# Moving a group of on-chip tiles by some hundred bytes in a fused attention, MLP and mixture-of-experts kernel

## The chip, the cores and the metric

The kernel runs on one core of a Trainium2 chip. The metric is the device time of one execution in microseconds (us). The engines are named as in the profile: PE is TensorE (matmul), PEld its weight loads, DVE is VectorE, ACT is ScalarE, POOL is GpSimd, and SP is SyncE, which issues most transfers.

## The reference, cut to what matters

Three stages follow one another. Sizes: 8 batches, 8 heads, 512 rows and 32 state rows of 64 values per head; so 8 x 544 = 4352 tokens of 512 values reach the MLP.

```python
def _attn_ref(x, state):                       # x (8, 8, 512, 64), state (8, 8, 32, 64)
    a = softmax(scale * x @ state.T)           # rows read the state
    xread = a @ state
    a2 = softmax(scale * state @ x.T)          # the state reads the rows
    sread = a2 @ x
    return concat([xread, sread], axis=2)

def _moe_ref(x, w_in, w_out):                  # (512, 2048), (2048, 512)
    h = x @ w_in
    return (h * clip(h + 3, 0, 6) / 6) @ w_out

def _moe2_ref(x, w_gate, w_output_gate, w1, w2):   # 8 experts, 512 -> 1024 -> 512
    e = argmax(x @ w_gate); gate = softmax(x @ w_gate)[e]
    eom = sigmoid(x @ w_output_gate)[e]
    out = gate * eom * (relu(x @ w1[e]) @ w2[e])   # each token by its one expert
```

## The kernel before, in words

Matmuls keep close to fp32 precision by three products: each operand is split into a high part of type fp32r (ScalarE copies it) and the rest (VectorE subtracts), and high x high, high x low and low x high are summed.

First half, until about 680 us. For each of eight batches, a block runs 16 steps of the MLP: L837 makes one 128 x 512 tile of the hidden layer from the attention weights (`att1_hi`, `att1_lo`, in the profile `att_hi` and `att_lo`) and a product of state and `w_in` that is made beforehand (`mix`); ScalarE and VectorE apply the activation; L855 multiplies by `w_out`, whose output stays in four PSUM banks. Between these steps stand the attention of the next batch (L776 scores, L785 transposes, L796 the read of `xb` with the weights `att2_t`) and the choice of expert of the batch before it; tables written out by hand (`ATT`, `POST`, `MIX`) fix their places. Rows are scattered to a bucket of their expert in HBM. A ninth, shorter block does the state's tokens (L827).

Second half. A loop goes over tiles of 128 rows from the buckets: rows are loaded to `xg`, turned by VectorE to `xg_raw` and split to `xg_t`; L912 multiplies by `w1`; ScalarE puts the result in `expert_hid`, which is written to `hidden` in HBM (L601) and read back in another order to `hid_mv` (L609), turned and split to `act_t`; L928 multiplies by `w2`; VectorE scales the result into `yo`, and GpSimd scatters it to the output (L691). When the expert changes, the next expert's raw weights, 2 MB each, which ScalarE's queue loads to `raw1` and `raw2` (L1119, L1125), are split into the half of `we` that isn't in use (L1076 on ScalarE, L483 on VectorE). The order of work on each engine is fixed by the program; waits are on semaphores.

Memory is laid out by hand. `at(name, offset, shape, dtype)` places a tile at `SBUF_BASE + offset` bytes of every partition, with `SBUF_BASE = 16512`. A running offset `o` is increased after each group, and many tiles lie over others whose time has passed. The order, from offset 131072 on, is: `mix` (16384 bytes), `hid_hi` with its followers and `att1_lo` (16384), `rows` at 163840, `keys0` (2048), `xb` (8192), `x_t` with `att2_t` (8192), then `late_at`: `sc1` (4096), `att1_hi` (4096), `att2` (4096), `sread` (4096), `keys1` (2048), `wg`, `ident`, two constants of type bf16, and then small tiles. In the second half the first 131072 bytes hold `we`, 131072 holds `raw2`, 147456 `act_t`, 163840 `xg` and `hid_mv` (over `rows`), and these lie behind it:

```python
    raw1_at = 163840 + ROWS_SIZE + 2048
    raw1 = at("raw1", raw1_at, [P, KD * F], F32)
    assert raw1_at + KD * F * 4 == late_at
    expert_hid = at("expert_hid", late_at, [P, F], F32)
    xg_t = [at(f"xg_t_{n}", late_at + 8192 + i * 4096, [P, 2, KD, P], F32R) for i, n in enumerate(("hi", "lo"))]
    yo = [at("yo0", raw1_at - 2048, [P, DM], F32), at("yo1", st_diag_at, [P, DM], F32)]
```

`st_diag_at` is the offset of `keys1`. P is 128 and BANK is 512; `rows` has CH x ROW = 4 x 516 values of 4 bytes a partition, 8256 bytes.

Of the kernel before, what the change touches and what calls it, by code (L numbers as in the profile page):

```python
# [25 lines left out]
F32 = mybir.dt.float32  # L26
# [7 lines left out]
P = 128  # L34
BANK = 512
# [4 lines left out]
def emit_kernel(nc, x_rows, x_t_dram, keys, w_in, w_out, gates, w1, w2, out):  # L40
# [4 lines left out]
    E = w1.shape[0]  # L45
    F = w1.shape[3]
    SCALE = float(D) ** -0.5
    KD = DM // P
    KF = FF // P
    KE = F // P  # L50
    CH = S // P
# [8 lines left out]
    ROW = DM + 4  # L60
# [16 lines left out]
    def at(name, offset, shape, dtype):  # L77
        return nc.alloc_sbuf_tensor_at(name, shape, dtype, offset=SBUF_BASE + offset)
# [4 lines left out]
    o = 131072  # L83
# [21 lines left out]

    x_t_second = at("x_t_second", 65536 + 2 * GO * DM * 4, [P, PAIRS, S], F32)

    ROWS_SIZE = -(-CH * ROW * 4 // BANK) * BANK
    o += ROWS_SIZE

    half_b = B // 2
# [30 lines left out]
    keys_s.append(at("keys1", o, [P, half_b, PAIRS, NS], F32))  # L142
    o += 2048

    wg = at("wg", o, [P, KD, 4 * E], F32)
    o += 512
    ident = at("ident", o, [P, P], F32)
    o += 512
    before = at("before", o, [P, P], BF16)
# [5 lines left out]
    def sb(name, shape, dtype=F32):  # L155
        n = 1
        for s in shape[1:]:
            n *= s
        size = -(-n * (2 if dtype == BF16 else 4) // 32) * 32
        small[0] += size  # L160
        assert small[0] <= 212832, small[0]
        return at(name, small[0] - size, shape, dtype)
# [90 lines left out]
    gate_s = sb("gate_s", [P, RING, ROW - DM])  # L253
    raw1_at = 163840 + ROWS_SIZE + 2048
    raw1 = at("raw1", raw1_at, [P, KD * F], F32)
# [1387 lines left out]
```

## Time and profile before

| | us |
|---|---|
| three runs | 1160.65, 1162.46, 1165.16 |
| median | 1162.46 |
| the profiled execution | 1165.16 |
| its span, first to last instruction | 1163.3 |
| mean granted TensorE clock, of full speed | 0.985 |

The profile is of one execution. Busy time of an engine is the time in which it had an instruction under way. The chain that ended last is followed back from the last instruction, at each step to what released it. In the windows view a DMA share of 1.00 means that all 16 DMA engines were busy throughout.

### The profile page before, as it was taken

To read this page: it belongs to the slowest core of one execution; us is meant where nothing else is said; L and a number is where in the kernel's file an instruction comes from. 1 tells how busy PE (TensorE), PEld (TensorE's weight loads), DVE (VectorE), ACT (ScalarE), POOL (GpSimd) and SP (SyncE) were. 2 spreads that over 40 slices of the span, in tenths; PEclk is the share of its full clock that TensorE was granted. 3 is DMA by queue.
4 is the path that set the end of the run, shared out by engine and by line. 5 is a ranking of instruction groups with operands and counts; after the bars stand their busy time and mean duration, and the time that the engine had idled before them with its cause. 6 is when DMAs were issued, how large, how long until landed. Compare 5 with 4: busy or idle time off the path is not lost.

```text
span 1163.3 us, 20895 instructions
## 1 busy us (share of the span) xinstructions
PE 1121.6 (96%) x6358; PEld 887.2 (76%) x6359; DVE 639.1 (55%) x1247; ACT 467.1 (40%) x780; POOL 77.0 (7%) x96
## 2 busy tenths in 40 slices
PE   9999999999999999999999988989999999979995
PEld 7777777777777777777778977767888888858884
DVE  6675654655646556556564347546474445556632
ACT  4554434443444344434544351425343223344420
POOL 0000100101001001010010110010110010101111
PEclk9999999999999999999999989999999999989998
DMA  9210111102101111020020275667675444847542
GB/s 366 90 37 7 67 37 37 43 32 74 37 6 69 37 37 41 33 74 1 1 110 1 101 245 179 217 237 233 203 248 180 153 145 130 282 149 215 161 139 65
DMA packets 98783, 131.36 MB, mean 113 GB/s; under 512 B 13967, under 2 KB 75023, under 8 KB 94352
## 3 DMA queue, kind: packets, MB, share of 16 engines
q1 hardware_dynamic: 91360, 89.35, 24.3%
q10 hardware_dynamic: 1584, 23.07, 5.5%
q0 software_dynamic: 5760, 17.90, 4.0%
q8 instruction: 47, 0.77, 0.3%
q14 instruction: 32, 0.26, 0.1%
HBM read 85.86 MB, written 45.47 MB: 113 GB/s over the span
## 4 chain that ended last, share of the span: by engine, by line
PE 85%; DVE 4%; DMA 3%; issue 3%; ACTq 2%; ACT 1%; SPq 1%; DVEq 0%; POOL 0%; POOLq 0%
PE y_ps L855 33%; PE h_ps L837 15%; PE y_ps L928 13%; PE y_ps L912 7%; PE h_ps L912 6%; PE a_ps L812 2%; PE h_ps L827 2%; DMA hidden<-expert_hid 1%; DMA hid_mv<-hidden 1%; ACTq L444 1%; DVE we L483 1%; PE a_ps L715 1%; PE a_ps L796 1%; SPq L609 1%; PE a_ps L776 1%
## 5 line engine op out<-in xcount | busy, mean ns | idle before, releaser
L855 PE MATMUL y_ps<-w_out_hi,hid_hi 128*128 128x512 f32 x544 | 217.6, 400 | 0.0
L855 PE MATMUL y_ps<-w_out_hi,hid_lo 128*128 128x512 f32 x544 | 212.2, 390 | 0.0
L855 PE MATMUL y_ps<-w_out_lo,hid_hi 128*128 128x512 f32 x544 | 212.0, 390 | 0.0
L928 PE MATMUL y_ps<-we,act_t_hi 128*128 (+1 forms) x608 | 189.0, 392 | 6.2 <-DVE act_t_lo L1559 3.6
L1365 DVE SCALAR_TENSOR_TENSOR hid<-hid,h_ps 128x512 f32<-128x512 f32 (+1 forms) x144 | 94.5, 656 | 166.3 <-ACT hid L1035 164.7
L837 PE MATMUL h_ps<-att_hi,mix 128*128 128x512 f32 x512 | 184.0, 402 | 0.1
L1035 ACT ACTIVATE hid<-h_ps,three 128x512 f32<-128x512 f32 (+1 forms) x144 | 95.5, 663 | 174.8 <-PE h_ps L837 151.4
L855 PEld LDWEIGHTS y_ps<-w_out_hi,hid_hi 128*128 128x128 f32 x544 | 102.1, 188 | 49.9 <-issue 30.4
L928 PEld LDWEIGHTS y_ps<-we,act_t_hi 128*128 128x128 f32 x608 | 114.6, 189 | 31.9 <-issue 8.2
L1374 DVE TENSOR_TENSOR hid_lo<-hid,hid_hi 128x512 fp32r<-128x512 f32 (+1 forms) x144 | 94.9, 659 | 70.5 <-ACT hid_hi L1043 69.5
L1552 DVE STREAM_TRANSPOSE act_raw<-hid_mv 128x512 f32<-128x512 f32 x76 | 49.5, 690 | 136.2 <-DMA hid_mv<-hidden 134.8
L855 PEld LDWEIGHTS y_ps<-w_out_hi,hid_lo 128*128 128x128 f32 x544 | 102.1, 188 | 22.3
L928 PE MATMUL y_ps<-we,act_t_lo 128*128 (+1 forms) x304 | 118.8, 391 | 0.0
L855 PEld LDWEIGHTS y_ps<-w_out_lo,hid_hi 128*128 128x128 f32 x544 | 102.3, 188 | 19.6
L837 PEld LDWEIGHTS h_ps<-att_hi,mix 128*128 128x128 f32 x512 | 96.1, 188 | 27.4 <-issue 7.0
L1043 ACT ACTIVATE hid_hi<-hid 128x512 fp32r<-128x512 f32 (+1 forms) x144 | 87.4, 607 | 67.0 <-DVE hid L1365 66.8
L912 PE MATMUL h_ps<-we,xg_t_hi 128*128 (+1 forms) x304 | 96.1, 398 | 9.9 <-DVE we L483 8.2
L912 PE MATMUL y_ps<-we,xg_t_hi 128*128 x304 | 95.2, 395 | 8.8 <-DVE xg_t_lo L1419 8.8
L837 PE MATMUL h_ps<-att_lo,mix 128*128 128x512 f32 x256 | 99.9, 390 | 0.0
L483 DVE TENSOR_TENSOR we<-raw,we 128x1024 f32 (+1 forms) x55 | 63.9, 1220 | 30.9 <-ACT we L1076 30.7
L1113 ACT ACTIVATE act_t_hi<-act_raw 128x512 fp32r<-128x512 f32 x76 | 45.8, 630 | 84.2 <-DVE act_raw L1552 84.1
L912 PEld LDWEIGHTS h_ps<-we,xg_t_hi 128*128 128x128 f32 x304 | 58.2, 192 | 23.1 <-issue 11.0
(216 smaller groups left out, 1409.5 us busy)
## 6 DMA issues: line engine op xcount, KB each, us to landing
raw<-in_w ACTq DMA_DIRECT2D x11, 2048.0 KB, 8.4
hidden<-expert_hid SPq DMA_DIRECT2D x76, 256.0 KB
hid_mv<-hidden SPq DMA_DIRECT2D x152, 128.0 KB
xg<-buckets SPq DMA_DIRECT2D x164, 64.0 KB
xb<-in_x_rows SPq DMA_DIRECT2D x8, 1024.0 KB, 4.9
x_t<-in_x_t SPq DMA_DIRECT2D x7, 1024.0 KB, 4.9
buckets<-pad_row SPq DMA_DIRECT2D x8, 774.0 KB, 8.0
raw<-in_w SPq DMA_DIRECT2D x3, 2048.0 KB, 7.5
```

What stands on the lines that cost most here:

```text
L483: ins = eng.tensor_tensor(we[:, bass.ds(w_at + piece(w, i, LO), PIECE)], raw[:, i * PIECE:(i + 1) * PIECE], we[:, bass.ds(w_at + piece(w, ...
L812: i = pe.matmul(mix_bank(a, n, g)[NS * q:NS * q + NS, :], keys_of(a)[D * g:D * g + D, q, :], w_in_raw[D * g:D * g + D, q, mix_columns(n)], ...
L837: i = pe.matmul(h_ps[:, j % 2, 0:cols], mix[:, m % SLOTS, g, n % GO, wp, :], (att1_hi, att1_lo)[tp][:, g, 0:cols], start=(g == 0 and k == ...
L855: i = pe.matmul(y_ps[:, t, :], (hid_hi, hid_lo)[hp][:, hid_at(b, j), t * P:(t + 1) * P], w_out_s[wp][:, j, :], start=(j == 0 and m == 0), ...
L912: i = pe.matmul(hid2_banks[slot % 2][:, h, :], xg_t[xp][:, slot % 2, k, :], we[:, bass.ds(w_at + (wp * WPART + k * F + h * BANK), BANK)], ...
L928: i = pe.matmul(y2_ps[:, slot % 2, :], act_t[hp][:, slot % 2, f, :], we[:, bass.ds(w_at + (wp * WPART + KD * F + f * DM), DM)], start=(f = ...
L1035: act.activation(hid[:, hid_at(b, j), 0:cols], h_ps[:, j % 2, 0:cols], ACT.Relu, bias=three).then_inc(sem("relu_ready"), 1)
L1043: act.activation(hid_hi[:, hid_at(b, j), 0:cols], hid[:, hid_at(b, j), 0:cols], ACT.Copy).then_inc(sem("hid_hi_ready"), 1)
L1113: act.activation(act_t[HI][:, slot % 2, h * 4:h * 4 + 4, :], act_raw[:, slot % 2, h * 4:h * 4 + 4, :], ACT.Copy).then_inc(sem("act_t_hi"), 1)
L1365: dve.scalar_tensor_tensor(out=hid[:, hid_at(b, j), 0:cols], in0=hid[:, hid_at(b, j), 0:cols], scalar=6.0, in1=h_ps[:, j % 2, 0:cols], op0 ...
L1374: dve.tensor_tensor(hid_lo[:, hid_at(b, j), 0:cols], hid[:, hid_at(b, j), 0:cols], hid_hi[:, hid_at(b, j), 0:cols].bitcast(F32), ALU.subtr ...
L1552: dve.transpose(act_raw[:, slot % 2, h * 4:h * 4 + 4, :].rearrange("p f t -> p (f t)"), hid_mv[:, h, :, :].rearrange("p s (k f) -> p k s f ...
```

## The change

The room behind `rows` is rounded up to a multiple of 128 bytes, 8320, where it was rounded to a multiple of 512, 8704. `wg` is placed 512 bytes further from the running offset, and the offset behind it grows by 1024 where it grew by 512. No instruction, loop, wait or transfer is added, taken away or put in another order.

```diff
-    ROWS_SIZE = -(-CH * ROW * 4 // BANK) * BANK
+    ROWS_SIZE = -(-CH * ROW * 4 // P) * P
     o += ROWS_SIZE
...
-    wg = at("wg", o, [P, KD, 4 * E], F32)
-    o += 512
+    wg = at("wg", o + 512, [P, KD, 4 * E], F32)
+    o += 1024
     ident = at("ident", o, [P, P], F32)
```

## Rows read from the trace of the kernel before

**Rows 1.** Part 1 of the page: busy us, share of the span, instructions.

```profile
PE 1121.6 (96%) x6358; PEld 887.2 (76%) x6359; DVE 639.1 (55%) x1247; ACT 467.1 (40%) x780; POOL 77.0 (7%) x96
```

**Rows 2.** Part 4 of the page: the chain that ended last, by engine.

```profile
PE 85%; DVE 4%; DMA 3%; issue 3%; ACTq 2%; ACT 1%; SPq 1%; DVEq 0%; POOL 0%; POOLq 0%
```

**Rows 3.** Windows of stages: busy us and count, granted clock, DMA share, GB/s.

```profile
60.00:600.00 540.00, 540.00 (x3312) 407.18 (x3311) 314.00 (x659) 238.86 (x417) 27.88 (x28) 1.00 0.12 41
...
695.00:830.00 135.00, 120.97 (x621) 99.41 (x620) 78.98 (x147) 48.11 (x71) 9.88 (x10) 0.96 0.66 213
830.00:985.00 155.00, 155.00 (x686) 128.38 (x685) 76.19 (x126) 51.59 (x83) 13.70 (x15) 1.00 0.56 175
985.00:1030.00 45.00, 36.78 (x156) 30.04 (x155) 28.97 (x41) 18.77 (x26) 3.90 (x4) 0.92 0.64 211
```

**Rows 4.** The chain in order of time (start us, us, what): start and busy stages.

```profile
1.05 5.54 PE h_ps L876 x60
...
93.03 2.96 PE y_ps L855 x12
95.99 2.72 PE h_ps L837 x12
100.96 2.72 PE y_ps L855 x12
...
822.61 5.44 PE h_ps L912 x24
828.05 5.44 PE y_ps L928 x24
```

**Rows 5.** The chain in order of time, around two changes of expert.

```profile
by line: PE y_ps L855 32.6%; PE h_ps L837 15.2%; PE y_ps L928 13.1%; PE y_ps L912 7.2%; PE h_ps L912 6.4%; issue 2.6%; PE a_ps L812 2.5%; PE h_ps L827 2.0%; DMA hidden<-expert_hid 1.5%; DMA hid_mv<-hidden 1.3%; ACTq L444 1.2%; DVE we L483 1
...
752.48 0.35 ACTq L1119
...
759.10 0.34 ACTq L1125
...
762.43 9.52 DMA hidden<-expert_hid
...
1002.24 0.34 ACTq L1125
...
1005.37 7.42 DMA hidden<-expert_hid
```

**Rows 6.** Windows of single transfers: x_t, raw1, expert_hid out (850 to 852), hid_mv (854).

```profile
466.50:467.00 0.50, 0.50 (x4) 0.42 (x3) 0.50 (x1) 0.00 (x0) 0.00 (x0) 1.00 1.03 426
467.00:467.50 0.50, 0.50 (x4) 0.42 (x3) 0.14 (x1) 0.32 (x1) 0.00 (x0) 1.00 0.97 410
...
584.00:585.00 1.00, 1.00 (x6) 0.83 (x5) 1.00 (x2) 1.00 (x3) 0.00 (x0) 1.00 0.99 426
585.00:586.00 1.00, 1.00 (x6) 0.84 (x5) 1.00 (x3) 0.27 (x1) 0.00 (x0) 1.00 1.07 459
...
850.00:851.00 1.00, 1.00 (x6) 0.81 (x5) 1.00 (x4) 0.44 (x1) 0.00 (x0) 1.00 0.70 262
851.00:852.00 1.00, 1.00 (x6) 0.84 (x5) 1.00 (x2) 0.00 (x0) 0.00 (x0) 1.00 0.68 258
...
854.00:855.00 1.00, 1.00 (x6) 0.84 (x5) 0.58 (x1) 0.00 (x0) 0.00 (x0) 1.00 1.06 358
```

**Rows 7.** Instructions of L796 and L837: ns least/median/most, first and last start us.

```profile
L796 PEld LDWEIGHTS a_ps<-xb,att_t x512: 106/110/110, 42.2 to 541.6; 128*32 128x32 f32 x171
L796 PE MATMUL a_ps<-xb,att_t x512: 219/219/243, 42.2 to 541.6; 128*32 128x64 f32 x171
...
L837 PE MATMUL h_ps<-att_hi,mix x512: 388/389/499, 18.7 to 625.5; 128*128 128x512 f32 x171
...
L837 PE MATMUL h_ps<-att_lo,mix x256: 387/389/398, 19.0 to 625.3; 128*128 128x512 f32 x128
```

## The prediction

> **What bounds the kernel now.** I read the page's busy shares first, then the chain that ended last, then windows of single stages. TensorE is busy 96% of the span and VectorE, the next one, 55% [rows 1]; the chain gives TensorE 85% of the span, DMA 3% [rows 2]. The windows show that these are two different regimes: from 60 to 600 us and from 830 to 985 us TensorE has no idle time at all, while around two changes of expert it does: 135 - 120.97 = 14.0 us idle between 695 and 830 us, and 45 - 36.78 = 8.2 us between 985 and 1030 us [rows 3]. In the busy stages the chain is a run of matmuls at an even pitch: 12 in 2.72 us in the first half, 24 in 5.44 us in the second, 227 ns each in both [rows 4]. So a change matters if it alters that pitch, or if it alters the transfers that the chain runs through at the changes of expert [rows 5].
>
> **What the edit moves.** It changes addresses alone: the same instructions in the same order with the same waits, bytes and semaphores. The sum over removed and added instructions is therefore 0 and what is left is whether an address has a price. `rows` takes 8256 bytes a partition; its room shrinks from 8704 to 8320, so everything from `keys0` to `keys1` moves down by 384 bytes. `wg` then gets a hole of 512 bytes ahead of it, so that it and all behind it move up by 128. Start addresses: `keys0` goes from 16512 + 163840 + 8704 = 189056, which is 738 x 256 + 128, to 188672 = 737 x 256. `wg` goes from 225920 (882 x 256 + 128) to 226048 = 883 x 256. Before, every large tile starts 128 bytes past a multiple of 256. After, those ahead of and including `rows` still do, and those behind it start on a multiple of 256. Aliased tiles keep their places relative to one another: `raw1` still ends at `late_at`, and `xg` with `hid_mv` (8192 bytes) still end ahead of `yo0`, 128 bytes away where it was 512. No new overlap, hence no new wait.
>
> **Its parts.** (1) Transfers with a moved end: the loads of `x_t`, `xb`, `keys`, `wg` and `raw1`, the writes of `expert_hid` to HBM, and the stores of `yo`. The other end is in HBM and stays. `raw2`, `xg`, `hid_mv` and the scattered `rows` stay. (2) TensorE operands that move: `att1_hi` (streamed by 512 matmuls on the chain of the first half), `xg_t` (only as weights), and the small ones `x_t`, `xb`, `att2_t`, `ident`, `wg`. All operands of L855 and L928, the largest groups, stay. (3) Operands of VectorE and ScalarE in the attention and in the split of `w1`.
>
> Part 1, from the DMA windows. Bandwidth divided by the busy share is what the 16 DMA engines reach when all are busy. The load of `raw1` (runs of 16 KB a partition) reaches 426/0.99 = 430 and 459/1.07 = 429 GB/s; the load of `x_t` (runs of 8 KB) 426/1.03 = 414 and 410/0.97 = 423; the write of `expert_hid` (runs of 2 KB) 262/0.70 = 374 and 258/0.68 = 379; a stretch of mostly 512-byte runs 358/1.06 = 338 [rows 6]. With 377 GB/s a 2 KB run takes 2048 / (377/16) = 87 ns of one engine, with 430 a 16 KB run takes 610 ns. A line through both has 0.0365 ns a byte and 12 ns fixed per run. Whatever a misplaced start costs per run is inside those 12 ns. If all of it vanished, 2 KB runs would be 14% faster and 16 KB runs 2%. That is the bound of the gain. Where is it exposed? The chain has 1.5% on the writes of `hidden`, and two pieces of it, 9.52 and 7.42 us, hold 16.9 us [rows 5]. 14% of 16.9 is 2.4 us. These pieces are far longer than 256 KB need (about 0.7 us at 377 GB/s): just before each, ScalarE's queue has issued the 2 MB load of `raw2` (L1125, at 759.10 and 1002.24), and before the first also that of `raw1` (L1119, at 752.48) [rows 5]. At 430 GB/s 2 MB take 4.9 us, so most of both pieces is the time of a load whose place is not changed (`raw2`) or can gain 2% (`raw1`, 0.1 us). What really belongs to `expert_hid` are its two writes of 0.7 us: 14% of 1.4 us is 0.2. So 2.4 is generous, and 0.3 us is nearer. The loads of `x_t` and `xb` inside the blocks lie under a TensorE without idle time [rows 3], and the first load of `x_t` lies under the 60 warm-up matmuls on which the chain stands until 6.59 us [rows 4]. Nothing. Stores of `yo` lie behind the matmuls until the very last, one of 256 KB: 14% of 0.7 us is 0.1. Part 1: between -2.5 us and 0, taken as -0.3.
>
> [...] No run here shows aligned runs yet.
>
> Part 2. The nearest rows are those where one line already starts at different residues. In L796 the weights are 32-column slices of `att2_t`, 128 bytes apart, so the 512 loads start 128, 256, 384 and 0 bytes past a multiple of 512 in turn. They take 106/110/110 ns (least, median, most). The streamed slices of `xb` are 256 bytes apart and take 219 ns at least and in the median [rows 7]. So the whole spread that an address could hide there is 4 ns. `att1_hi` and `att1_lo` both take 389 ns in the median in L837 [rows 7]. After the change they start at different residues. At 4 ns for each of the 512 matmuls on `att1_hi` the bound is 2.0 us lost; the same 4 ns the other way would be 2.0 gained, but the pitch of 227 ns is shared by forms with every kind of operand [rows 4], so I see nothing to gain. I take 0. Weight loads of `xg_t` run beside the matmuls (PEld 76% where PE has 96% [rows 1]) and would lie under them even 4 ns longer.
>
> Part 3. VectorE at 55% and ScalarE at 40% [rows 1] are not on the chain in the busy stages; at the changes of expert they are, with some dozens of instructions whose addresses partly moved. By the same 4 ns that is under 0.5 us either way. I take 0.
>
> **Sum.** The profiled execution took 1165.16 us, 1163.3 of span and 1.9 around it; with -0.3 it would take 1164.9. It was the slowest of three, 2.7 above the median of 1162.46. On the median: 1162.2 us. The bounds of the terms give -3.0 to +2.5.
>
> **Rivals.** A: start addresses matter to the DMA engines, and the changes of expert shorten. For it speak the chain's 16.9 us on `hidden` and the fixed part per run; against it that 16 KB runs already move at 430 GB/s from the old address, and that the same stalls hold waits on ScalarE and VectorE which don't move. At its bound it gives 1162.5 - 2.5 = 1160.0 us. To be faster by 0.5% (5.8 us) it would have to take a third off those 16.9 us, more than the 12 ns allow, unless a shorter transfer also gets a hidden write ahead of a 2 MB load; one such step, 7.42 us, would give 1155.0. B, the other side: TensorE reads `att1_hi` more slowly once it stands at another residue than the tiles that the other engines use at that time. Its place is L837 in the eight blocks, with no idle time under it to absorb it. For it speaks only that today all large tiles share one residue, so the trace can't show a mixture of them; against it the even spreads of L796, where slices at all four residues mix. It decides from 5.8 us / 512 = 11 ns a matmul, 5% of the pitch; at 15 ns it gives 1162.5 + 7.7 = 1170.2 us. C: a change of expert falls otherwise by chance, as transfers and queues shift by some tenths, and a stall grows or shrinks by one or two us. It gives 1160.5 to 1164.5, on either side.
>
> **Chances.** Within 0.5% (about what a measurement of this kernel can tell from no change; 1156.6 to 1168.3 us) lie my forecast at 0.68, C at 0.14 and A at or under its bound at 0.08: 0.90. A with a step ahead of a load, beyond 0.5%: 0.05. B beyond its threshold: 0.05. The range takes the lowest and highest of the three runs, 1160.65 and 1165.16, and adds the bounds of the terms, -3.0 and +2.5: 1157.6 to 1167.7.
>
> **What would show it.** Right: 12 matmuls of L837 still 2.72 us, both its forms at 389 ns, the write of `expert_hid` still near 377 GB/s at full share, the same instruction counts, the same idle time at the two changes of expert within 2 us. A: that rate at 400 or above and the pieces on `hidden` shorter. B: `att_hi` matmuls above `att_lo` and blocks longer than before. Wrong altogether: any group of VectorE or ScalarE whose mean moved by more than some ns.

## The result, and the profile after

Nine runs of each kernel: before 1165.16 us in the median (1160.65 to 1167.40), after 1172.17 us. The ratio is 1.0064, with a 95% interval of 1.0042 to 1.0087: slower by 7.5 us. One run of the changed kernel, 1598 us at a granted clock of 0.65, is left out of the ratio as disturbed; the other eight lie between 1167.90 and 1178.61. Four more executions of the changed kernel, the profiled one among them, took 1167.76, 1170.40, 1171.91 and 1173.89 us. The forecast was no change, 1162.2 us in a range up to 1167.7. The measured time lies above it. Of the 10.0 us between forecast and median, 2.7 are not the change: the kernel before had 1162.46 us in the median of its first three runs and 1165.16 in that of nine.

Order, counts, waits and transfers of the two kernels are the same, instruction for instruction. First the page of the changed kernel, its span, part 1 and the chain by engine, beside [rows 1, 2]:

```profile
span 1166.0 us, 20895 instructions
...
PE 1127.7 (97%) x6358; PEld 886.0 (76%) x6359; DVE 639.4 (55%) x1247; ACT 466.8 (40%) x780; POOL 76.8 (7%) x96
...
PE 85%; DVE 4%; issue 3%; DMA 2%; SPq 2%; ACTq 2%; ACT 1%; DVEq 0%; POOL 0%; POOLq 0%
```

VectorE, ScalarE and GpSimd are within 0.3 us of before. TensorE is busy 1127.7 - 1121.6 = 6.1 us longer with the same 6358 matmuls. That is the first hint: the work costs more where nothing waits. Then the chain of the changed kernel in order of time (start us, us, what), beside [rows 4]:

```profile
96.25 2.75 PE h_ps L837 x12
...
101.25 2.75 PE y_ps L855 x12
...
174.39 2.75 PE h_ps L837 x12
...
252.52 2.75 PE h_ps L837 x12
...
811.34 5.84 PE y_ps L912 x24
...
861.38 5.46 PE y_ps L928 x24
866.84 5.59 PE h_ps L912 x24
872.43 5.46 PE y_ps L928 x24
877.89 5.59 PE y_ps L912 x24
...
988.35 5.60 PE y_ps L912 x24
```

24 matmuls of L912 take 5.59 us where they took 5.44, (5.59 - 5.44)/24 = 6.2 ns each. 24 of L928 take 5.46, hardly more. In the first half, a block lasts 252.52 - 174.39 = 78.13 us; before, the same two groups stood at 173.71 and 251.45, 77.74 us apart. In [rows 4] 12 matmuls of L837 took 2.72 us where they now take 2.75, and so did 12 of L855, although both operands of L855 stand where they stood. The granted clock is 1.00 in both kernels from 60 to 600 us and from 830 to 985 us, so it isn't the clock. One step closer, the timeline of single matmuls in one L912 group after the change:

```profile
866.68 0.64 PE L912 MATMUL h_ps<-we,xg_t_hi 128*128 x2
867.15 0.39 PE L912 MATMUL h_ps<-we,xg_t_lo 128*128 x1
867.38 0.62 PE L912 MATMUL h_ps<-we,xg_t_hi 128*128 x2
867.84 0.39 PE L912 MATMUL h_ps<-we,xg_t_lo 128*128 x1
868.07 0.64 PE L912 MATMUL h_ps<-we,xg_t_hi 128*128 x2
```

and the same group before:

```profile
865.96 0.62 PE L912 MATMUL h_ps<-we,xg_t_hi 128*128 x2
866.42 0.39 PE L912 MATMUL h_ps<-we,xg_t_lo 128*128 x1
866.64 0.62 PE L912 MATMUL h_ps<-we,xg_t_hi 128*128 x2
867.10 0.39 PE L912 MATMUL h_ps<-we,xg_t_lo 128*128 x1
867.32 0.62 PE L912 MATMUL h_ps<-we,xg_t_hi 128*128 x2
```

Six matmuls take 867.32 - 865.96 = 1.36 us before and 868.07 - 866.68 = 1.39 after. Nothing is idle between them. A matmul's duration is longer than the interval to the next start (389 against 227 ns before), so the records overlap. The durations moved too, by a little less: from 389 to 393 and 395 ns in the median for L912, and for `att_hi` in L837 from 389 to 393 while `att_lo` stayed at 388 to 389. The weight loads of both stayed at 188 ns. The interval between starts gives the whole cost.

Where the 7.5 us are, by these rows. 38 tiles with 24 matmuls of L912 and 24 of L928 give at most 38 x (0.15 + 0.02) = 6.5 us. The last group of the first half (L855 x18) starts at 683.90 us where it started at 680.77, 3.1 us later. Together that is 9.6 us, of which some lies under other waits at the changes of expert. In the two profiled executions the spans differ by only 2.7 us, since the stretch from the last group of L855 to the first full run of L912 (from 680.77 to 811.46 before, from 683.90 to 811.34 after) was 3.2 us shorter in the execution of after; from there to the end it took 2.8 us longer, and 3.1 - 3.2 + 2.8 = 2.7. Over the kernels below that have this stall it lies between 126 and 132 us, whether `xg_t` is moved or not. So a span of one execution can't settle a half per cent here, while intervals of the even stretches repeat to 0.01 us (five blocks in a row at 77.74 us before and at 78.13 after). Such intervals, added up by line over five blocks of the first half, put 0.33 of the 0.39 us a block behind matmuls of L855 and 0.06 behind those of L837; no other line changes.

### The profile page after: what moved, and what is told of

The parts are those of the page before. It is cut to its first block, busy times and chain, and to the rows that moved or that the text cites. A ratio compares the mean times of both kernels' runs of the same rounds, so it can differ in the third digit from the quotient of the medians.

```text
span 1166.0 us, 20895 instructions
## 1 busy us (share of the span) xinstructions
PE 1127.7 (97%) x6358; PEld 886.0 (76%) x6359; DVE 639.4 (55%) x1247; ACT 466.8 (40%) x780; POOL 76.8 (7%) x96
## 4 chain that ended last, share of the span: by engine, by line
PE 85%; DVE 4%; issue 3%; DMA 2%; SPq 2%; ACTq 2%; ACT 1%; DVEq 0%; POOL 0%; POOLq 0%
PE y_ps L855 33%; PE h_ps L837 15%; PE y_ps L928 13%; PE y_ps L912 7%; PE h_ps L912 6%; PE a_ps L812 2%; PE h_ps L827 2%; DMA hid_mv<-hidden 1%; ACTq L444 1%; DVE we L483 1%; PE a_ps L715 1%; PE a_ps L796 1%; PE a_ps L776 1%; DMA hidden<-expert_hid 1%; SPq L574 1%
## 5 line engine op out<-in xcount | busy, mean ns | idle before, releaser
L855 PE MATMUL y_ps<-w_out_hi,hid_hi 128*128 128x512 f32 x544 | 218.6, 402 | 0.0
L855 PE MATMUL y_ps<-w_out_lo,hid_hi 128*128 128x512 f32 x544 | 213.0, 392 | 0.0
L855 PE MATMUL y_ps<-w_out_hi,hid_lo 128*128 128x512 f32 x544 | 212.6, 391 | 0.0
L928 PE MATMUL y_ps<-we,act_t_hi 128*128 (+1 forms) x608 | 187.9, 390 | 4.4 <-issue 2.6
L837 PE MATMUL h_ps<-att_hi,mix 128*128 128x512 f32 x512 | 184.5, 403 | 0.1
L855 PEld LDWEIGHTS y_ps<-w_out_hi,hid_hi 128*128 128x128 f32 x544 | 102.1, 188 | 51.1 <-issue 30.4
L928 PEld LDWEIGHTS y_ps<-we,act_t_hi 128*128 128x128 f32 x608 | 113.9, 188 | 30.3 <-issue 6.1
L855 PEld LDWEIGHTS y_ps<-w_out_hi,hid_lo 128*128 128x128 f32 x544 | 102.2, 188 | 23.2
L928 PE MATMUL y_ps<-we,act_t_lo 128*128 (+1 forms) x304 | 118.6, 390 | 0.0
L855 PEld LDWEIGHTS y_ps<-w_out_lo,hid_hi 128*128 128x128 f32 x544 | 102.3, 188 | 20.0
L837 PEld LDWEIGHTS h_ps<-att_hi,mix 128*128 128x128 f32 x512 | 96.1, 188 | 27.8 <-issue 7.0
L912 PE MATMUL h_ps<-we,xg_t_hi 128*128 (+1 forms) x304 | 97.1, 401 | 8.6 <-DVE we L483 7.6
L912 PE MATMUL y_ps<-we,xg_t_hi 128*128 x304 | 96.9, 400 | 8.4 <-DVE xg_t_lo L1419 8.4
L837 PE MATMUL h_ps<-att_lo,mix 128*128 128x512 f32 x256 | 99.9, 390 | 0.0
L912 PEld LDWEIGHTS h_ps<-we,xg_t_hi 128*128 128x128 f32 x304 | 57.8, 191 | 23.0 <-issue 9.8
```

Source lines behind the costliest of these rows:

```text
L837: i = pe.matmul(h_ps[:, j % 2, 0:cols], mix[:, m % SLOTS, g, n % GO, wp, :], (att1_hi, att1_lo)[tp][:, g, 0:cols], start=(g == 0 and k == ...
L855: i = pe.matmul(y_ps[:, t, :], (hid_hi, hid_lo)[hp][:, hid_at(b, j), t * P:(t + 1) * P], w_out_s[wp][:, j, :], start=(j == 0 and m == 0), ...
L912: i = pe.matmul(hid2_banks[slot % 2][:, h, :], xg_t[xp][:, slot % 2, k, :], we[:, bass.ds(w_at + (wp * WPART + k * F + h * BANK), BANK)], ...
L928: i = pe.matmul(y2_ps[:, slot % 2, :], act_t[hp][:, slot % 2, f, :], we[:, bass.ds(w_at + (wp * WPART + KD * F + f * DM), DM)], start=(f = ...
```

## The experiments

The theory that I formed from the trace, T: while one matmul streams its moving operand, the weights of the next are loaded. The rows show the overlap: in the kernel before, the weights of the matmul that starts at 866.64 us load from 866.42 on, 188 ns long, and the matmul ahead of it starts at 866.42 too. By T, if the two start at the same address modulo some power of two, matmuls follow one another in 227 ns; if not, they take some ns more. Before the change all large tiles started 128 past a multiple of 256, so they always agreed (were in step). Afterwards `xg_t` (weights of L912) and `att1_hi` (streamed in L837) start on a multiple of 256, and their partners `we` and `mix` don't. That the two disturb each other while one streams and the other loads is my assumption behind T, which no trace here shows directly; the experiments below test the agreement of the starts. The ratios below are each to the kernel before on the same chip, with their 95% interval.

**One part of the change alone.** `keys0` to `keys1` move, `wg` and the small tiles don't.

```diff
-    ROWS_SIZE = -(-CH * ROW * 4 // BANK) * BANK
+    ROWS_SIZE = -(-CH * ROW * 4 // P) * P
-    wg = at("wg", o, [P, KD, 4 * E], F32)
-    o += 512
+    wg = at("wg", o + 384, [P, KD, 4 * E], F32)
+    o += 512 + 384
```

> Only keys0 to keys1 (with xg_t, att1_hi, expert_hid, raw1) move down by 384 bytes; wg, ident and all small tiles stand where they stood before the change. Theory T (a matmul is slowed when the weights that load and the operand that streams start at different residues of the address): all of the change's loss comes from this part, so 24 matmuls of L912 take 5.59 us instead of 5.44, L928 stays near 5.44 to 5.46, a block of the first half takes 78.1 us instead of 77.7, and the time is 1.005 to 1.008 of before. Rival W (the loss comes from wg, ident, ones and the small tiles): 24 of L912 in 5.44 us, time within 0.2% of before.

Measured: ratio 1.0048 (1.0031 to 1.0065). L912 at 5.59 us, L928 at 5.46, two groups of L837 at 174.54 and 252.68 us, 78.14 apart. The intervals are those of the whole change, so W falls: `wg`, `ident` and the small tiles aren't the cause. The ratio ends just below what was expected; its interval overlaps with that of the whole change.

**One tile alone, `xg_t`.** All else stays, `yo1` and a scratch tile excepted, which have to give way.

```diff
-    xg_t = [at(f"xg_t_{n}", late_at + 8192 + i * 4096, ...
+    xg_t = [at(f"xg_t_{n}", late_at + 8192 + 128 + i * 4096, ...
-    xg_raw = at("xg_raw", late_at + 12288, [P, 2, KD, P], F32)
+    xg_raw = at("xg_raw", late_at + 12288 + 128, [P, 2, KD, P], F32)
...
-    ... at("yo1", st_diag_at, [P, DM], F32)]
+    ... at("yo1", st_diag_at + 128, [P, DM], F32)]
-    passed = at("passed", sread_at + 2048, [P, MT, E], F32)
+    passed = at("passed", sread_at + 2048 + 128, [P, MT, E], F32)
```

> The kernel before with xg_t alone (and yo1 and a scratch tile behind it) moved up by 128 bytes; the first half is untouched. Theory T: 24 matmuls of L912 take 5.59 us, the blocks of the first half keep 77.7 us, the time is 38 tiles x 24 x 6.2 ns = 5.7 us more, less what the changes of expert hide: ratio 1.003 to 1.005. Rival D (the loss comes from transfers with a moved end, raw1 and expert_hid, which stay here): L912 at 5.44 us, ratio 1.000.

Measured: ratio 1.0032 (1.0016 to 1.0048), 3.7 us. The chain of this kernel:

```profile
173.17 2.72 PE h_ps L837 x12
...
250.91 2.72 PE h_ps L837 x12
...
854.49 5.59 PE y_ps L912 x24
860.08 5.46 PE y_ps L928 x24
865.54 5.59 PE h_ps L912 x24
```

The first half is as before (250.91 - 173.17 = 77.74) and the second as after the change. The transfers of `raw1` and `expert_hid` are untouched here, so D falls. Another rival is left, the writes into `xg_t` by ScalarE and VectorE, which moved along with it. Against it speaks that all 24 matmuls of a group are slower and the next 24, of L928, with other weights, hardly are; in the next experiment `xg_t` is written at the same shifted place and nothing is slower.

**Everything moved by the same 128 bytes.**

```diff
-    SBUF_BASE = 16512
+    SBUF_BASE = 16512 + 128
```

> Every tile moves up by 128 bytes, so all start on a multiple of 256 and all residues are equal again. Theory T (only the difference between weights and streamed operand counts): 24 of L912 in 5.44 us, blocks of 77.7 us, ratio 1.000. Rival A (the absolute place counts, and starts on a multiple of 256 are slow for TensorE): L912 at 5.59 or more, and L855, L837 and L928 slower too, ratio 1.007 or more.

Measured: ratio 1.0006 (0.9985 to 1.0026), no difference. Its chain:

```profile
173.50 2.72 PE h_ps L837 x12
...
251.24 2.72 PE h_ps L837 x12
...
857.50 5.44 PE y_ps L928 x24
862.94 5.44 PE h_ps L912 x24
```

`xg_t` and `att1_hi` start on a multiple of 256 as in the changed kernel, and nothing is slower: A falls. What counts is not where a tile starts but whether its partner starts likewise.

**The first half.** `att1_hi` and all behind it up by 128 bytes (the added line shifts the line numbers in its rows by one):

```diff
+    o += 128
     att1_hi = at("att1_hi", o, [P, GROUPS, S], F32R)
```

> The kernel before with att1_hi and all that lies behind it in the first half (att2, sread, keys1, wg, ident, small tiles) moved up by 128 bytes, while sc1, x_t, xb, raw1, expert_hid and xg_t stay. Theory T: L912 stays at 5.44 us for 24, since xg_t stays; the streamed att1_hi of L837 now differs from mix, so blocks of the first half take about 78.1 us instead of 77.7, 3 us in all: ratio 1.002 to 1.003. Rival (the first half is slowed by x_t, xb or att2_t): blocks of 77.7 us, ratio 1.000.

Measured: ratio 1.0023 (1.0007 to 1.0039), 2.7 us.

```profile
174.38 2.75 PE h_ps L838 x12
...
252.52 2.75 PE h_ps L838 x12
...
858.58 5.44 PE y_ps L913 x24
```

252.52 - 174.38 = 78.14 us a block, as after the change, and L912 as before. Then the same without `att1_hi`:

```diff
     att1_hi = at("att1_hi", o, [P, GROUPS, S], F32R)
-    o += 4096
+    o += 4096 + 128
```

> The kernel before with the tiles behind att1_hi (att2, sread, keys1, wg, ident, small tiles) moved up by 128 bytes while att1_hi stays. Theory T, which lays the slower first half to the streamed att1_hi alone: blocks of 77.7 us, ratio 1.000. Rival: one of the others costs, blocks near 78.1 us as when all of them moved together.

Measured: ratio 1.0003 (0.9983 to 1.0024); two groups of L837 at 173.70 and 251.48 us, 77.78 apart, and 77.75 in later blocks. Of 0.40 us a block, 0.36 or more go with `att1_hi`; the other tiles account for 0.01 to 0.04. Which of them it is was not tried. What goes with `att1_hi` is mostly the slower L855: with `att1_hi` moved, the matmuls of L855 hold 0.34 us a block more than before and those of L837 0.06; with it in place 0.02 more and 0.01 less.

**How far apart?** The second experiment with other distances, one run each, read by the interval alone (in the diff above 32, 64, 256 and 512 in place of 128).

> The kernel before with xg_t (and yo1 and a scratch tile) moved by 32 bytes alone. If any difference between the residues of weights and streamed operand costs, 24 matmuls of L912 take about 5.59 us as with 128 bytes; if the cost grows with the distance, between 5.44 and 5.59; if only steps of 128 or 256 bytes count, 5.44.

> The same with 64 bytes: 5.59 us for 24 of L912 if any difference costs, between 5.44 and 5.59 if the cost grows with distance, 5.44 if only 128 bytes and more count.

> The same with 256 bytes: 5.44 us for 24 of L912 if the address counts modulo 256, 5.59 or more if it counts modulo 512 or over.

> The same with 512 bytes, the control for moving xg_t at all: 5.44 us for 24 of L912 if the address counts modulo 512 or less; 5.59 would mean that it counts modulo more than that, or that the distance between tiles and not the residue is what costs.

The chain with 32 bytes:

```profile
856.05 5.59 PE y_ps L912 x24
861.64 5.45 PE y_ps L928 x24
```

with 64 bytes:

```profile
853.60 5.60 PE y_ps L912 x24
859.20 5.47 PE y_ps L928 x24
```

and with 256 bytes:

```profile
856.92 5.44 PE y_ps L928 x24
862.37 5.44 PE h_ps L912 x24
```

With 512 bytes L912 is at 5.44 too. So 32, 64 and 128 bytes cost alike, and 256 and 512 nothing: among these distances the start counts modulo 256, and the cost is whole at the smallest one. Their single times were 1172.3, 1169.2, 1163.5 and 1163.0 us beside 1169.4 for the kernel before; with one run each they prove nothing by themselves.

**Out of the changed kernel.** First `xg_t` moved back into step (the diff of the second experiment, with 384 in place of 128, on the changed kernel), then all of the late tiles:

> The changed kernel with xg_t (and yo1 and a scratch tile) alone moved up by 384 bytes, so that it stands 128 past a multiple of 256 like we. Theory T: 24 of L912 back to 5.44 us, blocks of the first half still 78.1 us, ratio to before 1.003. Rival (another moved tile of the second half, expert_hid or raw1, costs as well): ratio 1.005 or more.

```diff
     o += 8192
+    o += 384
     late_at = o
...
-    wg = at("wg", o + 512, [P, KD, 4 * E], F32)
-    o += 1024
+    wg = at("wg", o + 128, [P, KD, 4 * E], F32)
+    o += 640
...
-    raw1_at = 163840 + ROWS_SIZE + 2048
+    raw1_at = 163840 + ROWS_SIZE + 384 + 2048
```

> The changed kernel with all from late_at to keys1 and raw1 back where they stood before; only keys0, xb, x_t with att2_t (down by 384) and wg, ident and the small tiles (up by 128) stay moved. Theory T: blocks of 77.7 us, 24 of L912 in 5.44 us, ratio 1.000. Rival (the small operands x_t, xb, att2_t, ident cost in the first half): blocks over 77.8 us, ratio 1.001 or more.

Measured: with `xg_t` back, ratio 1.0024 (1.0006 to 1.0041), L912 at 5.44 us and blocks of 252.89 - 174.75 = 78.14 us, so only the first half's loss is left. With all late tiles back, ratio 1.0006 (0.9987 to 1.0025), L912 at 5.44 us, and two groups of L837 at 174.22 and 251.98 us, 77.76 apart. The tiles that stay moved there, `x_t`, `xb`, `att2_t`, `ident` and the small ones, cost 0.02 us a block.

**The cost enlarged on purpose.** `hid_hi` and `hid_lo`, the weights of all 1632 matmuls of L855, are put out of step with `w_out`, and `att1_lo`, which 256 matmuls of L837 stream, with `mix`:

```diff
+    o += 128
     hid_hi = at("hid_hi", o, [P, HRING, S], F32R)
...
-    o += ROWS_SIZE
+    o += ROWS_SIZE - 128
```

> The largest group is put out of step on purpose: hid_hi and hid_lo (weights of all 1632 matmuls of L855), att1_lo and rows move up by 128 bytes, w_out and all else stay. Theory T: about 6 ns more for each matmul of L855, less the 1.3 ns that it already loses on average, so 1632 x 5 ns = 8 us more, blocks near 78.7 us, L912 at 5.44 us for 24, ratio 1.007. Rival (only L912 and L837 are sensitive, for a reason of their own such as their loops): blocks under 78.0 us.

Measured: ratio 1.0074 (1.0046 to 1.0103), 8.6 us.

```profile
175.58 2.79 PE h_ps L838 x12
...
254.37 2.79 PE h_ps L838 x12
...
859.99 5.44 PE y_ps L913 x24
```

254.37 - 175.58 = 78.79 us a block, near the forecast, with L912 at 5.44. It is no property of L912 or L837: the three pairs tried, of L912, L837 and L855, all pay. The forecast had left out `att1_lo`, though. By the intervals between starts, 0.82 of the 1.05 us more in a block stand behind L855 and 0.23 behind L837. At 6.2 ns for each of the 192 matmuls of L855 and 32 on `att1_lo` in a block it would be 1.39 us, so in this mixture one costs 4.7 ns on average. That the total came near 8 us is in part luck.

No run was faster than the kernel before beyond its interval, and since its large tiles are all in step, the experiments point to no better version by this means.

## Why the prediction was wrong, point by point

- **What bounds the kernel: right.** TensorE's even pitch sets the time of most stages, and the change came out as a change of that pitch: 227 to 233 ns in L912.
- **Part 1, the transfers, -0.3 us with a bound of -2.5: no gain shows in the time.** The load of `raw1` in the changed kernel, in the windows view beside [rows 6]:

```profile
587.00:588.00 1.00, 1.00 (x6) 0.83 (x5) 1.00 (x3) 1.00 (x2) 0.00 (x0) 1.00 1.07 459
588.00:589.00 1.00, 1.00 (x6) 0.81 (x5) 1.00 (x2) 0.00 (x0) 0.00 (x0) 1.00 0.99 426
```

  459/1.07 = 429 and 426/0.99 = 430 GB/s are the rates of before to the digit, from a start on a multiple of 256. For the 2 KB runs of `expert_hid` the packets' own durations in the traces tell more than a window. In the ten traces where that tile starts 128 past a multiple of 256, its 9728 packets take 85.3 to 85.7 ns in the mean, and 57 to 65% of them take 84 ns or less. In the four where it starts on a multiple of 256 they take 84.2 to 84.5 ns, and 97 to 98% take 84 or less. So part 1 had the right side: from a start on a multiple of 256 a packet took about 1.2 ns less of 85.5, 1.4% where the bound was 14%. Over 16 engines that is 9728 x 1.2 / 16 = 730 ns of transfer time in all, mostly beside a busy TensorE, and the ratio doesn't show it: kernels with and without that tile moved are both at 1.0006. The idle time of TensorE at the two changes of expert was 13.2 and 7.6 us after, 14.0 and 8.2 before, within the 2 us that the prediction allowed.
- **Part 2, the operands of TensorE, 0 with a bound of 2.0 us: the step that failed.** It had two faults. The price of a mixture was read from L796 [rows 7], where half of the weight slices do start at another place than the streamed ones, and the spread is 4 ns. But L796 is another shape, 64 columns where L837 and L912 stream 512, and its rows read 110 and 219 ns after the change as before; they say nothing on what the long matmuls pay. For those the trace had no row out of step. The first half lost 8 x 0.39 = 3.1 us, nearly all of it with `att1_hi`: 6.1 ns for each of its 512 matmuls, where 0 was taken and 4 ns was the bound. And the weight loads of `xg_t` were set to nothing because they "would lie under" the matmuls. They do lie under them, at an unchanged 188 ns, and yet each matmul that uses them costs 6.2 ns more: 912 matmuls, 5.7 us, the larger part of the loss. The bound of 2.0 us covered `att1_hi` alone.
- **Part 3, VectorE and ScalarE at 0: right,** 639.1 to 639.4 and 467.1 to 466.8 us busy.
- **Rival B had the right side and half the place.** It named `att1_hi` at another residue than the rest. Both of its signs came: `att_hi` at 393 ns above `att_lo` at 388, and longer blocks. That is real and costs 0.36 us a block, under 3 us, less than its threshold of 5.8; it named the other engines' tiles as the partner where it is TensorE's own second operand, and it left out `xg_t`. With 0.05 its chance was too low: the text said itself that the trace could not show a mixture, and an unknown of that kind on the resource that bounds 85% of the chain deserved a wider bound than 4 ns.
- **Rival A fell as a cause of the time,** and C is seen in single executions, where stretches of changes of expert differ by several us, but not in the ratio.

The slower matmuls of L855 in the changed kernel, whose own operands hadn't moved, go with `att1_hi`, as the experiments on the first half show. They hold most of its cost. How it gets there is argued from intervals: after an interruption the matmuls run unevenly even in step, and then fall into 227 ns. The second half shows it after a stall: the first 24 of L912 took 5.71 us at 811.46 us before, against 5.44 for the next ones. So do the 45 runs of 12 matmuls of L855 that stand behind the attention: by their place in the run, the second to tenth interval is 227.1 to 234.6 ns in the mean in the kernel before and 227.6 to 234.0 in the changed one. In 65 other runs L855 comes in 12 behind 6 of L837. There the first eleven intervals are 226.6 to 227.8 ns in the kernel before; in the changed one the first nine are 227.3 to 233.4, and the next two are at 227. Behind L912 the same tail is shorter: leaving out intervals above 300 ns, the first three of L928 are 228.6, 232.1 and 230.8 ns in the mean in the changed kernel, then 227. So a group out of step slows the matmuls behind it until they are back at the even pitch, and in a run of 12 that takes nearly all of it.

Which of two starts must agree isn't settled. By T it is the streamed operand and the weights of the next matmul, which load meanwhile. The last experiment speaks for it: from the last `att_hi` of L837, whose own operands agree, to the first of L855, whose weights don't, the mean interval is 233.0 ns against 228.8 before, while from the last of L855 to L837, where the next weights agree, it is 228.4 against 226.7. But in the changed kernel the first of these intervals should be slow by T as well, and it is 227.1. What happens inside the chip, why 256 bytes apart costs nothing and 128 does, and why the cost is the same for 32 as for 128, stays open.

## What to carry to other kernels

Where a kernel lives off back-to-back matmuls (here fp32r, 128 x 128 weights, 512 columns), place weights and streamed operands with the same start address modulo 256 bytes (227 against 233 ns a matmul in L912); moving a single tile by 32 bytes cost 2.7% of the pitch of all matmuls that load from it. Read such a cost from the length of a long run of matmuls in the chain (24 in 5.59 or 5.44 us) rather than from the duration of one, where it is 4 to 6 ns in 389, and look for it also in the group behind. And when every tile of a trace shares a property, the trace holds no evidence on what it costs to break it: an edit that breaks it needs a wide bound on the engine that sets the time.

## What the runs showed of the hardware that I had not expected

- Weights and streamed operand of fp32r matmuls of 128 x 128 by 512 columns: 227 ns a matmul with equal starts modulo 256 bytes, 233 in L912 with starts 32, 64 or 128 bytes apart, and 227 again at 256 and 512.
- The effect spreads to the matmuls behind it: groups with equal starts that follow a group with unequal ones were slower too (24 of L928 at 5.46 us where they took 5.44; 12 of L855 at 2.75 where they took 2.72). In the first half this tail, 0.33 us a block, is larger than the cost in the group out of step itself, 0.06 us.
- A load of 2 MB in runs of 16 KB a partition reached 430 GB/s from a start 128 bytes past a multiple of 256 and from a multiple of 256 alike.
- Writes to HBM in 2 KB runs: 84.2 to 84.5 ns a packet in the mean from a start on a multiple of 256 bytes (four traces), 85.3 to 85.7 from 128 past one (ten traces).
